# Attention's product with v in plain fp32 on two column halves of the array, with one copy of the turned probabilities

## The chip, the cores and the metric

The kernel runs on one core of one Trainium2 chip. What is measured is the time of the device for one execution, in microseconds (us). TensorE (PE in the profile) multiplies; its weight loads are listed apart as PEld. VectorE is DVE, ScalarE is ACT, GpSimd is POOL, and SyncE (SP) issues nearly all of the transfers.

## The reference

Three stages follow each other. The change is in the first.

```python
# attention: q, k, v are (4, 8, 576, 64); blocks of 64, a block sees itself and what is before it
scores = 1.0 / np.sqrt(D) * np.matmul(q, k.transpose(0, 1, 3, 2))
scores = np.where(block_i >= block_j, scores, -1000000000.0)
attn = np.exp(scores - np.max(scores, axis=-1, keepdims=True))
attn = attn / (np.sum(attn, axis=-1, keepdims=True) + 1e-09)
x = np.matmul(attn, v)                      # then as (2304, 512)
# first feed-forward: w_in (512, 2048), w_out (2048, 512)
h = x @ w_in
x = np.maximum(0.01 * h, h) @ w_out
# second: a skip score, 8 experts, each token to its best expert
y[mask] = gate_w[mask, None] * (np.maximum(xc[mask] @ w1[e], 0.0) @ w2[e])
out[do_compute] = xc + y
```

## The kernel before

**Numbers.** Most products are made of three matmuls in the type F32R: a value is split into a high part (a copy to F32R) and a low part (the value minus the high part), and high by high, high by low and low by high are added in PSUM. The products of the experts' first layer (L1431) and of the gate (L1369) are plain fp32 instead.

**Units and steps.** The 32 heads go in 16 pairs. A pair has 9 units: four query tiles of 128 rows of its first head, one unit with the last 64 rows of both heads (TAIL), four tiles of the second head. The tile number qt (0 to 3) has 128 x (qt + 1) key columns. There are 144 units and 156 steps (STEPS), and at each step s every engine does its part of some unit: PE the scores of unit s + 2 and the transposes of unit s - 2, DVE the row maximum of s, ACT the exponential of s, and ACT and DVE take the transposed probabilities of unit s - 3 out of PSUM. Each engine runs its list in order; all waits are semaphores.

**The path of the probabilities.** `transposes(u)` writes the probabilities, keys on partitions, to one of two banks of `ps_t`. `high_p` (L822 to L828) copies them on ACT to `pt_hi`, and `low_p` (L963 to L966) writes `pt_lo`, bank minus `pt_hi`, on DVE. The bank is free for unit u + 2 after that. Both tiles exist once, so `high_p` waits at some units for the products of the pair before (L825, L826).

**The products with v.** `p_v` (L1265 to L1288) multiplies v (weights, 128 keys by 128 columns) with the turned probabilities (moving, up to 320 query columns). `v_hi` and `v_lo` hold, for each head, its 64 columns beside 64 zero columns, so that the two heads' matmuls with full width add into the same bank `ps_o`, one head into partitions 0 to 63, the other into 64 to 127. Queries are cut in two halves: columns 0 to 255 (two key tiles) and 256 to 575 (five key tiles, the last with 64 rows). The table P_V gives the steps: for pair p at its step 8 and at steps 1, 3, 4, 5, 6 of the next pair. `high_v` on ACT and `low_v` on POOL split v, which is loaded to `v_raw`.

**The row sums.** After a pair, `invert` on DVE adds 1e-9 and takes the reciprocal, PE turns it (L1293), DVE copies it out (`copy_inverse`), SP stores it to memory and spreads it back (`store_inverse`, `spread_inverse`), and POOL multiplies (`normalise`) what `copy_o` took out of `ps_o`. Then ACT and POOL split the result into the input of the first feed-forward.

**Hidden work.** FILL puts groups of the first feed-forward's matmuls (`hidden(g)`, twelve of 384 columns each) behind PE's work of the steps from 50 on: 16 groups at steps 50 to 83, 32 at 86 to 119, 9 at 122 to 142, and the rest of 64 after step 148. From step 38 on SP also loads w_in.

**SP's list** per pair: at step 2 the loads of k and q of the second head of the next pair (6) and of v (2), at 3 a copy of k and the store of the inverse, at 5 the spreading of the inverse (3), at 6 the loads for a first head (4), at 7 a copy of k.

Of the kernel before, what the change touches and what calls it, by code (L numbers as in the profile page):

```python
# [15 lines left out]
P = 128  # L16
# [16 lines left out]
QT = 5  # L33
# [10 lines left out]
P_V = {8: (0, 0, 0, 6), 1: (1, 0, 0, 6), 3: (0, 1, 0, 8), 4: (0, 1, 8, 15), 5: (1, 1, 0, 8), 6: (1, 1, 8, 15)}  # L44
# [31 lines left out]
def fill_steps():  # L76

    at = {s: [] for s in range(STEPS)}
    for g in range(N_ATT_HID):
        if g < FC:  # L80
            at[50 + 34 * g // FC].append(g)
        elif g < 3 * FC:
            at[86 + 34 * (g - FC) // (2 * FC)].append(g)
        elif g < TWO_BANKS:
            at[122 + 5 * (g - 3 * FC) // 2].append(g)
        else:
            at[N_UNITS + 5 + g - TWO_BANKS].append(g)
    return at

# [28 lines left out]
def build(nc, q_t, k_t, v_r, w_in, w_out, w_gs, w1, w2, out):  # L118
    ctx = ExitStack()
    with ctx:  # L120
# [151 lines left out]
        s_v = sem("s_v")  # L272
# [5 lines left out]
        s_vhi = sem("s_vhi")  # L278
        s_vlo = sem("s_vlo")
# [4 lines left out]
        s_pthi = sem("s_pthi")  # L284
        s_ptlo = sem("s_ptlo")
# [59 lines left out]
        N_FULL, N_CONST = 7, 11  # L345
# [43 lines left out]
        def split_done(u):  # L389

            p, i = divmod(u, UNITS)
            return 10 * p + i + 1 + (i > TAIL)

        def pt_views(u):

            i = u % UNITS
            if i == TAIL:
                src = t_bank(u, P, 0, BANK).rearrange("p (k h q) -> p h k q", k=4, h=2)
                return [[src] + [t[:, :, PT_B:PT_W].rearrange("p h (k c) -> p h k c", k=4)[:, :, :, A_COLS:B_COLS]
                                 for t in (pt_hi, pt_lo)]]  # L400
            h, qt = (0, i) if i < TAIL else (1, i - TAIL - 1)
            if qt < 2:
                src = t_bank(u, P, 0, P * (qt + 1))
                views = [[src] + [t[:, h, P * qt:P * qt + P * (qt + 1)] for t in (pt_hi, pt_lo)]]
                if i == TAIL + 1:
                    src = t_bank(u, D, P, 2 * P).rearrange("p (h q) -> p h q", h=2)
                    views.append([src] + [t[0:D, :, TAIL_COL:TAIL_COL + D] for t in (pt_hi, pt_lo)])
                return views
            src = t_bank(u, P, 0, P * (qt + 1)).rearrange("p (k q) -> p k q", q=P)
            return [[src] + [t[:, h, PT_B:PT_W].rearrange("p (k c) -> p k c", k=4)[:, 0:qt + 1, P * (qt - 2):P * (qt - 1)]  # L410
                             for t in (pt_hi, pt_lo)]]


        V_PARTS = ((P, 0, QT - 1), (D, QT - 1, QT))
# [39 lines left out]
        def load_v(e, p):  # L454
            b, hp = p // KC, p % KC
            full = (QT - 1) * P
            if p >= 1:
                e.wait_ge(s_vlo, 2 * p)
            e.dma_start(v_raw[:, 0:QT - 1, :],
                        v_r[b, 0:full, hp * P:(hp + 1) * P].rearrange("(t p) c -> p t c", p=P)).then_inc(s_v, 16)  # L460
            e.dma_start(v_raw[0:D, QT - 1, :], v_r[b, full:S, hp * P:(hp + 1) * P]).then_inc(s_v, 16)
# [3 lines left out]
        def _(e):  # L465
# [75 lines left out]
            for s in range(STEPS):  # L541
                p, i = divmod(s, UNITS)
                if p < N_PAIRS:
                    if i == 2 and p + 1 < N_PAIRS:
                        load_head(e, 2 * p + 3)
                        load_v(e, p + 1)
                    if i == 3 and p + 1 < N_PAIRS:
                        copy_k(2 * p + 2)
                    if i == 6 and p + 2 < N_PAIRS:
# [12 lines left out]
                for g in FILL.get(s - 1, ()):  # L562
                    store_hidden(g)
            for g in FILL[STEPS - 1]:
                store_hidden(g)
            e.wait_ge(s_h, N_ATT_HID)
            e.wait_ge(s_pv, 4 * N_PAIRS)
# [40 lines left out]
        def _(e):  # L608
# [18 lines left out]
            for i in range(2):  # L627
                e.memset(v_hi[i][:, :, 1, :].bitcast(F32), 0.0).then_inc(s_const, 1)
                e.memset(v_lo[i][:, :, 1, :].bitcast(F32), 0.0).then_inc(s_const, 1)
            e.memset(ident[:, :], 0.0).then_inc(s_const, 1)  # L630
            e.wait_ge(s_const, N_FULL)
            for i in range(2):
                e.memset(q2[i][D:P, DM:QW].bitcast(F32), 0.0).then_inc(s_const, 1)
                e.memset(k2[i][D:P, DM:S].bitcast(F32), 0.0).then_inc(s_const, 1)

# [10 lines left out]

            def low_v(p):
                i = p % 2
                for n, (rows_, t0, t1) in enumerate(V_PARTS):
                    e.wait_ge(*before[0])  # L650
                    e.wait_ge(s_vhi, 2 * p + n + 1)
                    before[0] = s_vlo, 2 * p + n + 1
                    e.tensor_tensor(v_lo[i][0:rows_, t0:t1, 0:3:2, :],
                                    v_raw[0:rows_, t0:t1, :].rearrange("p t (g c) -> p t g c", g=2),
                                    v_hi[i][0:rows_, t0:t1, 0:3:2, :].bitcast(F32), ALU.subtract).then_inc(s_vlo, 1)
# [29 lines left out]
            low_v(0)  # L685
            for s in range(STEPS):
# [6 lines left out]
                if i == 2 and 1 <= p < N_PAIRS:  # L693
                    low_v(p)
                if i == 8 and 1 <= p <= N_PAIRS:
# [89 lines left out]
        def _(e):  # L785
# [16 lines left out]
            def high_v(p):  # L802
                i = p % 2
                e.wait_ge(s_v, 32 * (p + 1))
                if p >= 2:
                    e.wait_ge(s_pv, 4 * (p - 1))
                for rows_, t0, t1 in V_PARTS:
                    e.activation(v_hi[i][0:rows_, t0:t1, 0:3:2, :],
# [665 lines left out]
```

## Time and profile before

| | |
|---|---|
| median of three runs | 859.65 us (858.75 to 859.67) |
| profiled execution | 856.37 us, of which the trace spans 854.5 us |
| PE busy | 810.5 us, 95% |
| PEld busy | 736.9 us, 86% |
| DVE, ACT, POOL busy | 414.2, 359.7, 196.8 us |
| granted clock of TensorE, mean | 0.98 |

An engine is counted as busy from an instruction's start to its end, waits in its pipeline among it; matmuls overlap, so the distance from start to start says what one costs, and its duration does not. The attention stage ends at about 360 us.

### The profile page before, as it was taken

How to read it: one execution, taken by the hardware profiler on the slowest of the kernel's cores; microseconds unless marked ns; L12 is line 12 of the kernel's file. 1: busy time of each engine (PE TensorE's matmuls, PEld its weight loads, DVE VectorE, ACT ScalarE, POOL GpSimd, SP SyncE). 2: the span in 40 equal slices, each digit the busy share in tenths (PEclk: the TensorE clock that was granted, in tenths of full speed). 3: DMA queues.
4: the chain of work that ended last, by engine and by line, in shares of the span. 5: the costliest groups of instructions: out<-in, count | busy, mean ns of one | idle time of the engine just before them, and what ended most of it. 6: DMA issues, size and time to landing. Idle time of an engine off the chain costs nothing.

```text
span 854.5 us, 14147 instructions
## 1 busy us (share of the span) xinstructions
PE 810.5 (95%) x4885; PEld 736.9 (86%) x4885; DVE 414.2 (48%) x835; ACT 359.7 (42%) x850; POOL 196.8 (23%) x226
## 2 busy tenths in 40 slices
PE   4889999999999999999999999999999589999999
PEld 3778899999999999899998888888888489888887
DVE  4777766664334456402335455555553232344464
ACT  4677767665445566423442222221221031333353
POOL 5354666433213224110010000000000141221221
PEclk9999799999999999999999999999999879999999
DMA  6444466744453343136666655655561137577740
GB/s 149 132 122 136 142 186 195 203 126 141 118 146 112 105 137 105 50 98 193 173 180 182 190 148 172 182 180 145 168 186 50 38 113 248 174 216 233 227 135 3
DMA packets 101545, 126.82 MB, mean 148 GB/s; under 512 B 15986, under 2 KB 62210, under 8 KB 101480
## 3 DMA queue, kind: packets, MB, share of 16 engines
q1 hardware_dynamic: 98392, 121.33, 48.3%
q0 software_dynamic: 2000, 3.77, 1.4%
q10 hardware_dynamic: 1088, 0.89, 0.5%
q8 instruction: 37, 0.61, 0.3%
q14 instruction: 28, 0.23, 0.1%
HBM read 92.58 MB, written 31.57 MB: 145 GB/s over the span
## 4 chain that ended last, share of the span: by engine, by line
PE 89%; DVE 4%; issue 3%; ACT 3%; DMA 1%; POOL 0%; SPq 0%; DVEq 0%; ACTq 0%; POOLq 0%
PE ps_hid L1431 11%; PE ps_o L1286 9%; PE ps_h L1310 8%; PE ps_x L1345 8%; PE ps_x L1347 8%; PE ps_h L1312 8%; PE ps_h L1311 8%; PE ps_x L1346 8%; PE ps_t L1262 4%; PE ps_y L1442 3%; PE ps_y L1443 3%; PE ps_y L1444 3%; PE ps_s L1247 2%; PE ps_s L1248 2%; PE ps_s L1237 1%
## 5 line engine op out<-in xcount | busy, mean ns | idle before, releaser
L966 DVE TENSOR_TENSOR pt_lo<-ps_t,pt_hi 128x512 fp32r<-128x512 f32 (+4 forms) x160 | 76.5, 486 | 147.1 <-ACT pt_hi L828 146.8
L1310 PE MATMUL ps_h<-xh,win_h 128*128 128x384 f32 x384 | 132.8, 346 | 1.3 <-ACT act L839 1.0
L1311 PE MATMUL ps_h<-xl,win_h 128*128 128x384 f32 x384 | 128.8, 335 | 0.0
L1312 PE MATMUL ps_h<-xh,win_l 128*128 128x384 f32 x384 | 128.7, 335 | 0.0
L1345 PE MATMUL ps_x<-wout_h,g_hi 128*128 128x512 f32 x288 | 116.3, 404 | 0.0
L1347 PE MATMUL ps_x<-wout_h,g_lo 128*128 128x512 f32 x288 | 112.9, 392 | 0.0
L1346 PE MATMUL ps_x<-wout_l,g_hi 128*128 128x512 f32 x288 | 112.1, 389 | 0.0
L1431 PEld LDWEIGHTS ps_hid<-rows_t,w_sb 128*128 128x128 f32 x768 | 89.5, 196 | 8.8 <-issue 8.4
L1431 PE MATMUL ps_hid<-rows_t,w_sb 128*128 128x128 f32 x768 | 91.0, 281 | 5.1 <-PE ps_y L1444 4.2
L839 ACT ACTIVATE act<-ps_h 128x384 f32<-128x384 f32 x96 | 47.1, 491 | 110.1 <-PE ps_h L1312 108.4
L819 ACT ACTIVATE prob<-ps_s,neg_max 128x128 f32<-128x128 f32 (+2 forms) x144 | 78.9, 548 | 25.7 <-DVE neg_max L960 25.2
L828 ACT ACTIVATE pt_hi<-ps_t 128x512 fp32r<-128x512 f32 (+4 forms) x160 | 67.6, 434 | 50.3 <-PE ps_o L1286 31.4
L643 POOL TENSOR_TENSOR k_st<-k_raw,k_st 64x576 fp32r<-64x576 f32 x32 | 45.9, 1433 | 161.6 <-DVE k_st L946 151.1
L1262 PE MATMUL ps_t<-ident,prob 128*128 128x128 f32 x384 | 70.5, 288 | 5.3 <-DVE pt_lo L966 5.3
L1310 PEld LDWEIGHTS ps_h<-xh,win_h 128*128 128x128 f32 x384 | 72.1, 188 | 3.8 <-ACT act L839 1.7
L1003 DVE TENSOR_TENSOR g_lo<-g_raw,g_hi 128x512 fp32r<-128x512 f32 x72 | 49.5, 687 | 52.2 <-ACT g_hi L849 52.2
L960 DVE TENSOR_REDUCE neg_max<-ps_s 128x1 f32<-128x128 f32 (+2 forms) x144 | 72.4, 503 | 0.6 <-PE ps_s L1248 0.5
L1286 PE MATMUL ps_o<-pt_hi,v_hi 128*128 128x320 f32 (+3 forms) x224 | 69.6, 311 | 2.7 <-DVE o_f L988 2.7
L1311 PEld LDWEIGHTS ps_h<-xl,win_h 128*128 128x128 f32 x384 | 72.2, 188 | 0.0
L1312 PEld LDWEIGHTS ps_h<-xh,win_l 128*128 128x128 f32 x384 | 72.1, 188 | 0.0
L1286 PE MATMUL ps_o<-pt_hi,v_lo 128*128 128x320 f32 (+3 forms) x224 | 68.6, 306 | 0.0
L1286 PE MATMUL ps_o<-pt_lo,v_hi 128*128 128x320 f32 (+3 forms) x224 | 66.1, 295 | 0.0
(154 smaller groups left out, 1422.3 us busy)
## 6 DMA issues: line engine op xcount, KB each, us to landing
w_sb<-in_w SPq DMA_DIRECT2D x64, 512.0 KB, 5.2
hidden<-act SPq DMA_DIRECT2D x96, 192.0 KB, 2.2
g_raw<-hidden SPq DMA_DIRECT2D x72, 256.0 KB, 4.5
k_raw<-in_k_t SPq DMA_DIRECT2D x62, 144.0 KB, 2.9
q_raw<-in_q_t SPq DMA_DIRECT2D x32, 144.0 KB, 2.9
x2rows<-x SPq DMA_DIRECT2D x18, 256.0 KB, 2.4
out<-x SPq DMA_DIRECT2D x18, 256.0 KB, 2.6
k<-k_st SPq DMA_DIRECT2D x31, 144.0 KB, 2.7
```

The source lines that it names most:

```text
L819: e.activation(prob_of(u), score_out(u), ACT.Exp, bias=neg_max[:, u % 4:u % 4 + 1], scale=1.0, accum_out=row_sum[p % 2][:, i:i + 1]).then_ ...
L960: e.tensor_reduce(out=neg_max[:, u % 4:u % 4 + 1], in_=src, axis=AX.XY if u % UNITS == TAIL else AX.X, op=ALU.max, negate=True).then_inc(s ...
L966: e.tensor_tensor(lo, src, hi.bitcast(F32), ALU.subtract).then_inc(s_ptlo, 1)
L1262: last = e.transpose(t_bank(u, P, P * kt, P * kt + P), tile[:, P * kt:P * kt + P], ident[:, :])
L1286: last = e.matmul(ps_o[:, a:a + cols], stat, (pt_hi, pt_lo, pt_hi)[j][0:kr, h, at:at + cols], start=h == 0 and n == 0, stop=h == 1 and n = ...
L1310: e.matmul(dst, win_h[:, f, kc, :], xh[slot][:, kc, :], start=kc == 0, stop=False)
L1311: e.matmul(dst, win_h[:, f, kc, :], xl[slot][:, kc, :], start=False, stop=False)
L1312: last = e.matmul(dst, win_l[:, f, kc, :], xh[slot][:, kc, :], start=False, stop=kc == KC - 1)
L1345: e.matmul(dst, hi, wout_h[:, f, :], start=f == 0, stop=False)
L1346: e.matmul(dst, hi, wout_l[:, f, :], start=False, stop=False)
L1347: last = e.matmul(dst, lo, wout_h[:, f, :], start=False, stop=f == FC - 1)
L1431: last = e.matmul(ps_hid[half][:, P * f - HALF * half:P * (f + 1) - HALF * half], w1_sb[i][:, c, P * f:P * f + P], rows_t[:, c, :], start= ...
```

## The change

The two heads of a pair no longer share full-width matmuls with zero columns. Each product with v is one matmul in plain fp32 with 64 weight columns, the first head into partitions 0 to 63 of `ps_o`, the second into 64 to 127, one after the other for each key tile. v is used as it was loaded (`v_sb`, two buffers), and the splits `high_v` and `low_v` go. The turned probabilities are copied once, to `pt` (two buffers, one a pair), by ACT for units 3 and 8 of a pair and by DVE for the others. The last key tile uses all 128 rows; the unused ones are set to zero once.

With it: the products are at steps 1, 3 and 4 of the next pair (P_V has three entries, both heads in each); the transposes have a third bank, `ps_h1`, up to unit 44, before the first hidden group needs it; hidden groups are cut in two parts that FILL places apart; the second `copy_o` is at step 5 instead of 7, `normalise` at 7 instead of 8; SP issues the loads of v at step 5, ahead of the spreading; the addition of 1e-9 is on ACT (step 8); ACT's copy of a hidden group stands ahead of the exponential of the step.

```diff
-P_V = {8: (0, 0, 0, 6), 1: (1, 0, 0, 6), 3: (0, 1, 0, 8), 4: (0, 1, 8, 15), 5: (1, 1, 0, 8), 6: (1, 1, 8, 15)}
+P_V = {1: (0, 0, 2), 3: (1, 0, 2), 4: (1, 2, 5)}
+PT_ACT = (3, 8)
+T3_UNITS = 5 * UNITS
...
-        v_raw = sb("v_raw", [P, QT, P], F32, r2)
-        v_hi = [sb(f"v_hi{i}", [P, QT, 3, D], F32R, r2) for i in range(2)]
-        v_lo = [sb(f"v_lo{i}", [P, QT, 3, D], F32R, r2) for i in range(2)]
+        v_sb = [sb(f"v_sb{i}", [P, QT, P], F32, r2) for i in range(2)]
...
-        pt_hi = sb("pt_hi", [P, 2, PT_W], F32R, r2)
-        pt_lo = sb("pt_lo", [P, 2, PT_W], F32R, r2)
+        pt = [sb(f"pt{i}", [P, 2, PT_W], F32, r2) for i in range(2)]
...
         def t_bank(u, rows_, a, z):
-            c = BANK * (u % 2)
-            return ps_t[0:rows_, c + a:c + z]
+            n = t_index(u)
+            return ps_h1[0:rows_, a:z] if n == 2 else ps_t[0:rows_, BANK * n + a:BANK * n + z]
...
+        def turned_ready(e, u):
+            p = u // UNITS
+            e.wait_ge(s_ptr, u + 1)
+            if p >= 2:
+                e.wait_ge(s_pv, 2 * (p - 1))
...
         def load_v(e, p):
-            if p >= 1:
-                e.wait_ge(s_vlo, 2 * p)
+            if p >= 2:
+                e.wait_ge(s_pv, 2 * (p - 1))
...
                     if i == 2 and p + 1 < N_PAIRS:
                         load_head(e, 2 * p + 3)
-                        load_v(e, p + 1)
...
+                    if i == 5 and p + 1 < N_PAIRS:
+                        load_v(e, p + 1)
...
+            def add_epsilon(p):
+                rs = row_sum[p % 2]
+                e.wait_ge(s_exp, UNITS * (p + 1))
+                e.activation(rs[:, :], rs[:, :], ACT.Copy, bias=1e-9).then_inc(s_eps, 1)
...
-            def low_p(u):
-                e.wait_ge(s_pthi, split_done(u))
-                for src, hi, lo in pt_views(u):
-                    e.tensor_tensor(lo, src, hi.bitcast(F32), ALU.subtract).then_inc(s_ptlo, 1)
+            def copy_turned(u):
+                turned_ready(e, u)
+                for src, dst in pt_views(u):
+                    e.tensor_copy(dst, src).then_inc(s_ptd, 1)
...
+            def p_v(p, half, first, end):
                 if first == 0:
+                    turned(e, UNITS * p + (TAIL + 2, UNITS - 1)[half])
+                    e.wait_ge(s_v[p % 2], 32 * (p // 2 + 1))
+                    if p + half >= 1:
+                        e.wait_ge(s_of, 2 * p + half)
+                    if half:
+                        e.wait_ge(s_invt, p + 1)
...
-                    stat = (v_hi, v_hi, v_lo)[j][i][0:kr, kt, h:h + 2, :].rearrange("p g c -> p (g c)")
-                    last = e.matmul(ps_o[:, a:a + cols], stat, (pt_hi, pt_lo, pt_hi)[j][0:kr, h, at:at + cols],
-                                    start=h == 0 and n == 0, stop=h == 1 and n == len(steps) - 1)
+                    for h in range(2):
+                        own = slice(D * h, D * h + D)
+                        last = e.matmul(ps_o[own, a:a + cols], v_sb[p % 2][:, kt, own], pt[p % 2][:, h, at:at + cols],
+                                        start=kt == 0, stop=kt == tiles - 1)
```

## Rows read from the trace of the kernel before

**Rows 1.** Windows cut at L1293: us, then PE, PEld, DVE, ACT, POOL busy, clock, DMA.

```profile
28.90:45.60 16.70, 13.64 (x93) 11.77 (x93) 12.46 (x29) 11.60 (x34) 5.71 (x5) 1.00 0.45 126
45.60:62.30 16.70, 14.91 (x93) 13.27 (x93) 12.45 (x29) 11.60 (x34) 7.63 (x8) 0.90 0.45 125
...
79.00:96.80 17.80, 15.61 (x93) 13.35 (x92) 13.03 (x29) 12.59 (x36) 10.48 (x10) 0.86 0.60 171
96.80:118.70 21.90, 21.01 (x128) 19.91 (x129) 13.34 (x31) 15.53 (x44) 12.44 (x11) 0.88 0.58 165
...
238.60:268.30 29.70, 29.52 (x190) 28.53 (x190) 12.83 (x28) 15.43 (x43) 7.72 (x7) 1.00 0.43 124
```

**Rows 2.** Chain of waits, 45 to 63 us: start, us, engine, what.

```profile
46.54 0.77 PE ps_s L1237 x4
...
55.40 0.61 ACT pt_hi L828
...
61.06 0.90 DVE row_sum L971
```

**Rows 3.** Waits of the whole span: total us, times, longest us.

```profile
ACT pt_hi L828 <- PE ps_o L1286: 31.4, 29, 2.0
```

**Rows 4.** PE in order of time (start, us): from three bursts of products with v.

```profile
143.22 0.39 PE L1286 MATMUL ps_o<-pt_hi,v_hi 128*128 128x320 f32 x1
...
144.47 0.28 PE L1247 MATMUL ps_s<-k_st,q_hi 128*128 128x256 f32 x1
...
254.40 0.39 PE L1286 MATMUL ps_o<-pt_hi,v_lo 128*128 128x320 f32 x1
...
254.83 0.27 PE L1286 MATMUL ps_o<-pt_hi,v_lo 128*128 128x192 f32 x1
255.03 0.29 PE L1286 MATMUL ps_o<-pt_hi,v_hi 64*128 64x64 f32 x1
...
255.48 0.44 PE L1310 MATMUL ps_h<-xh,win_h 128*128 128x384 f32 x1
...
261.00 0.36 PE L1286 MATMUL ps_o<-pt_hi,v_hi 128*128 128x256 f32 x1
...
261.73 0.39 PE L1310 MATMUL ps_h<-xh,win_h 128*128 128x384 f32 x1
```

**Rows 5.** Plain fp32: L1431 on the page, and two stretches of PE's order.

```profile
L1431 PE MATMUL ps_hid<-rows_t,w_sb 128*128 128x128 f32 x768 | 91.0, 281 | 5.1 <-PE ps_y L1444 4.2
...
742.90 7.41 PE L1431 MATMUL ps_hid<-rows_t,w_sb 128*128 128x128 f32 x64 [0.58 <-PE ps_y L1444]
...
502.76 0.96 PE L1369 MATMUL ps_gate<-wg,x2t 128*128 128x9 f32 x8
```

**Rows 6.** Weight loads (PEld) of the same burst as 255.03 in rows 4.

```profile
255.03 0.18 PEld L1286 LDWEIGHTS ps_o<-pt_hi,v_hi 64*128 64x128 f32 x1
255.14 0.19 PEld L1286 LDWEIGHTS ps_o<-pt_lo,v_hi 64*128 64x128 f32 x1
```

**Rows 7.** PE around a transpose with 64 weight columns, and that one's load.

```profile
257.70 0.22 PE L1247 MATMUL ps_s<-k_st,q_hi 128*128 128x128 f32 x1
...
257.87 0.28 PE L1260 MATMUL ps_t<-ident,prob 128*64 128x128 f32 x1
...
257.83 0.11 PEld L1260 LDWEIGHTS ps_t<-ident,prob 128*64 128x64 f32 x1
```

**Rows 8.** Groups of ACT and DVE in 28.9 to 79 us: busy us, mean ns.

```profile
L828 ACT ACTIVATE pt_hi<-ps_t 128x512 fp32r<-128x512 f32 (+4 forms) x30 | 12.6, 430 | 6.4 <-PE ps_o L1286 4.5 <-PE ps_t L1262 1.6
...
L971 DVE TENSOR_SCALAR row_sum<-row_sum 128x9 f32<-128x9 f32 x3 | 2.9, 966 | 0.0
```

**Rows 9.** SP's issues in order of time around the store of an inverse.

```profile
49.32 0.58 SPq L468 DMA_DIRECT2D k<-k_st  x1
49.94 0.50 SPq L472 DMA_DIRECT2D inverse<-inv_t  x1
51.95 0.45 SPq L480 DMA_DIRECT2D inv_all<-inverse  x1
```

More of the change, by code:

```diff
@@ L79, in fill_steps, with filled_at, t_index, t_before @@
     for g in range(N_ATT_HID):
[L80 to L87, printed above, removed]
-    return at
+        for part in range(2):
+            n = 2 * g + part
+            if g < FC:
+                s = 50 + 34 * n // (2 * FC)
+            elif g < 3 * FC:
+                s = 86 + 34 * (g - FC) // (2 * FC)
+            elif g < TWO_BANKS:
+                s = 122 + 22 * (n - 6 * FC) // (2 * (TWO_BANKS - 3 * FC))
+            else:
+                s = N_UNITS + 5 + g - TWO_BANKS
+            at[s].append((g, part))
+    return at
+def filled_at(s):
+    return [g for g, part in FILL.get(s, ()) if part]
+def t_index(u):
+    return u % 3 if u < T3_UNITS else u % 2
+def t_before(u):
+    return next((v for v in range(u - 1, max(u - 4, -1), -1) if t_index(v) == t_index(u)), None)
 FILL = fill_steps()
@@ L271, in build @@
         s_qk = [sem(f"s_qk{i}") for i in range(2)]
-        s_v = sem("s_v")
+        s_v = [sem(f"s_v{i}") for i in range(2)]
         s_khi = sem("s_khi")
@@ L645, in low_k @@
                 before[0] = s_klo, n + 1
[L647 to L655, printed above, removed]
             def normalise(p):
@@ L684, in _ @@
             low_k(1)
-            low_v(0)
             for s in range(STEPS):
@@ L692, in _ @@
                         low_k(2 * p + 3)
-                if i == 2 and 1 <= p < N_PAIRS:
-                    low_v(p)
-                if i == 8 and 1 <= p <= N_PAIRS:
+                if i == 7 and 1 <= p <= N_PAIRS:
                     normalise(p - 1)
@@ L1014, in _ @@
                     maximum(s)
-                if 3 <= s < N_UNITS + 3:
-                    low_p(s - 3)
+                if 3 <= s < N_UNITS + 3 and (s - 3) % UNITS not in PT_ACT:
+                    copy_turned(s - 3)
                 if p + 1 < N_PAIRS:
@@ L1293, in turn_inverse, with hidden, hidden_waits @@
                 e.transpose(ps_o[0:UNITS, B_COLS:B_COLS + P], inv[:, :], ident[:, :]).then_inc(s_invp, 1)
-            def hidden(g):
+            def hidden(g, part):
                 m, f = divmod(g, FC)
                 slot = m % 4
+                dst = ps_hidden(g)
+                if part == 0:
+                    hidden_waits(g)
+                for kc in range(KC // 2 * part, KC // 2 * (part + 1)):
+                    e.matmul(dst, win_h[:, f, kc, :], xh[slot][:, kc, :], start=kc == 0, stop=False)
+                    e.matmul(dst, win_h[:, f, kc, :], xl[slot][:, kc, :], start=False, stop=False)
+                    last = e.matmul(dst, win_l[:, f, kc, :], xh[slot][:, kc, :], start=False, stop=kc == KC - 1)
+                if part:
+                    last.then_inc(s_h, 1)
+            def hidden_waits(g):
+                m, f = divmod(g, FC)
+                if g == 0:
+                    turned(e, T3_UNITS - 1)
                 if f == 0:
@@ L1307, in hidden @@
                     e.wait_ge(s_act, g)
-                dst = ps_hidden(g)
-                for kc in range(KC):
-                    e.matmul(dst, win_h[:, f, kc, :], xh[slot][:, kc, :], start=kc == 0, stop=False)
-                    e.matmul(dst, win_h[:, f, kc, :], xl[slot][:, kc, :], start=False, stop=False)
-                    last = e.matmul(dst, win_l[:, f, kc, :], xh[slot][:, kc, :], start=False, stop=kc == KC - 1)
-                last.then_inc(s_h, 1)
             scores(0)
@@ L1322, in _ @@
                 p, i = divmod(s, UNITS)
-                if i in P_V:
-                    pair = p if i == 8 else p - 1
-                    if 0 <= pair < N_PAIRS:
-                        p_v(pair, *P_V[i])
-                    if i == 1 and 1 <= p <= N_PAIRS:
-                        turn_inverse(pair)
-                for g in FILL[s]:
-                    hidden(g)
+                if i in P_V and 1 <= p <= N_PAIRS:
+                    p_v(p - 1, *P_V[i])
+                    if i == 1:
+                        turn_inverse(p - 1)
+                for g, part in FILL[s]:
+                    hidden(g, part)
             for g in range(N_ATT_HID, N_HID):
-                hidden(g)
+                for part in range(2):
+                    hidden(g, part)
             def project(k):
```

119 lines of the change are left out of this document (48 added, 71 removed).

## The prediction

> **What bounds the kernel now.** I read the windows table first, cut at the instruction of L1293 that turns a pair's inverse row sums (one per pair of heads). Pairs without hidden work inside them take 16.70 us, whether the granted clock is 1.00 or 0.90 [rows 1]; so TensorE's speed does not set them, although PE counts as busy for 13.6 to 14.9 us. A pair that also holds the first projection's matmuls (238.6 to 268.3 us) has PE busy for all but 0.2 us [rows 1]: there the order of PE's instructions is the time. The attention stage has two halves with different limits; the border is step 50 of 144.
>
> The chain of waits of one early pair shows the loop of the first half: the scores of the tail unit (46.54), then PE alone through the steps with four bursts of products with v until ACT's pt_hi copy at 55.40, then ACT and DVE to the end of row_sum at 61.96 and one maximum and exponential more [rows 2]. That is 8.8 us on PE and 7.9 on ACT and DVE, in series: 16.7. The wait in the middle exists because pt_hi is a single buffer; all waits of that kind come to 31.4 us [rows 3].
>
> **What the products with v cost now.** At full clock a burst of eight F32R products of 320 columns starts at 143.22 and the next instruction at 144.47: 1.25 us. The second kind (one product of 320, three of 192, three of 64) takes 254.40 to 255.48, 1.08 us; the short one 261.00 to 261.73, 0.73 us [rows 4]. A pair has each twice: 2 x 3.06 = 6.12 us. The hidden matmuls beside them are untouched (the same 64 groups, cut in halves).
>
> **The new products.** Over its seven key tiles a head has 384 + 960 + 192 + 64 = 1600 columns. Plain fp32 stands in the expert stage: a loop body has 32 such products (4 chunks by 8 blocks), the row says x64, so two records a product; 7.41 us less the last one's tail of 0.17 is 113 ns a record of 128 columns [rows 5]. Are that the weights or the columns? The gate's eight records of only 9 columns follow at (0.96 - 0.25) / 7 = 0.10 us [rows 5], so weights alone explain most of it, and 0.88 ns a column is only an upper bound; the lower is F32R's 1.25 us / (8 x 320) = 0.49 [rows 4]. I take 0.875: a 128-column F32R record whose weights are in lasts 0.22 us [rows 7], an fp32 one 0.281 [rows 5], longer by just another 128 columns at F32R's rate, so the columns pass twice. One head: 1600 x 2 x 0.875 = 2.8 us (1.6 at the lower bound).
>
> The heads now fill partitions 0 to 63 and 64 to 127 of ps_o from the two column halves of the array. No row shows two halves at work together, so I bound it. Side by side without loss: 2.8 us, and 0.7 us for the first record of each of three bursts, which has no partner: 3.5. In series: 5.6. Weights are loaded one ahead (255.14, under the matmul of 255.03 [rows 4, 6]), so a partner starts late by one small load, about 0.08 us (a 64-column load lasts 0.11 [rows 7]); 14 such offsets are 1.1 us. Then the change of shape. Where a burst goes from 128 rows to 64, the next matmul starts 0.20 us after the last instead of 0.11, and its load only then, at 255.03 [rows 4, 6]: a gap of 0.09 us, and another one back. The change removes all four of a pair, since the last key tile now uses 128 rows. The column change, in contrast, is free where it can be seen: the load for 64 columns starts at 257.83, under running matmuls, and its transpose 0.04 later [rows 7]. So six changes between full and half columns cost between 0 and 6 x 0.09 = 0.5 us. Bounds side by side: 3.5 to 5.1; I take the middle, 4.3, since neither row is nearer: a saving of 1.8 us a pair (1.0 to 2.6).
>
> The Trainium skill (TensorEngine Tiling (Array Packing), Key Properties) says that changing the tiling mode drains the engine. The trace agrees for 64 rows (0.09 us) and disagrees for the 64-column transposes; the sum would be 0.25 us a pair worse or better by the one or the other.
>
> **Second half, steps 55 to 144.** 9.9 pairs bound by PE: 9.9 x 1.8 = 17.8 us. Waits of ACT for the single pt_hi buffer (31.4 us in all, 1.5 in each early pair [rows 3, 8]) are mostly hidden here; I give 2 us for them. Sum 20. DVE and ACT stay cover: busy 12.8 and 15.4 of 29.7 us [rows 1]. Halving a hidden group adds no instruction; its copy moves ahead of the exponential on ACT, which PE needs only two steps later.
>
> **First half, steps 0 to 55.** What leaves ACT: ten pt_hi copies, 4.2 us a pair [rows 8], of which two of 0.6 stay, and v_hi. What leaves DVE: ten subtractions become eight copies (0.69 each for the two of 512 that leave; I price a copy like the subtraction, since both read the same bank), and row_sum's addition, 0.97 a pair [rows 8], goes to ACT. POOL loses low_v. New floors of a pair:
> - DVE: 12.45 [rows 1] - 1.4 - 1.0 = 10.1.
> - PE's issue: scores 3.7, 25 transposes x 0.11 = 2.8, products 4.3: 10.8 (12.6 before).
> - SP: an issue comes 0.62 us after another [rows 9]; 18 of them (10 for q and k, 2 for v, 2 copies of k, 1 + 3 of the inverse) are 11.2. It also stands from 50.44 to 51.95 until the inverse has landed [rows 9]; load_v moves into exactly that place and covers 1.2 of the 1.5. Floor 11.5. load_v's new wait, for the products of the pair before last, is over by then; behind it are the spreading and the loads of q and k.
> - The loop of [rows 2], redone: from the tail scores PE goes through two bursts instead of four (1.3 + 0.4 + 0.4 + 1.4 + 0.6 + 0.9, 5.0), then comes o_f's second copy, moved from step 7 to 5, and DVE's steps 5 to 10, some 5.8 us by the durations of its maxima, copies and q, then the exponential, 0.9: 11.7. The pt_hi waits go, through two buffers and the third transpose bank (up to unit 44). A new wait of PE, the second burst for inv_t (DVE, step 2), ends just before the o_f copy that it waits for anyway: 0; behind it stand the scores and transposes of the step after, due two steps later.
>
> Three limits of 11.7, 11.5 and 10.8 do not overlap perfectly; I take 12.6. Start to step 10, 18.1 us: -3.7. Three pairs: 3 x 4.1 = 12.3. 79.0 to 96.8, where SP also loads w_in (22.5 issues, 14.0): 17.8 to 14.6, -3.2. 96.8 to 118.7, with three hidden groups of 2.1 on PE (10.8 + 6.3, with friction 17.8): -4.1 [rows 1]. Sum 23.3; with 15.0 a pair 12, with 11.7 a pair 28.
>
> The start is not touched: transfers of q and k set it, not the memsets that are exchanged. The stages after attention hold the same instructions.
>
> **The sum.** 20 + 23.3 = 43.3. The profiled execution took 856.4 us, hence 813.1; the median of the runs is 3.3 us above it, hence 816.4.
>
> **Rivals.**
> - *The halves do not run together* (0.22). Products 5.6 + 0.5 = 6.1 a pair: the second half gains only its 2 us. In the first half PE issues 12.6 a pair and the loop is 11.7 + 1.6, with friction 14.3: 2 + 3 x 2.4 + 1.5 + 1.3 = 12. Time 859.65 - 14 = 846. For it: no row shows two products at once. Against: the next weights are taken under a running matmul everywhere, and the halves share neither weights nor columns nor partitions of ps_o; that puts it below the forecast. The Trainium skill (TensorE: Matmul & The Clock Gate, Part 3, Measured speedup vs the span model) gives 2.38x for three column tiles; no run here shows it.
> - *The products gain, the first half does not* (0.07): landings of SP's transfers hold early pairs at 15.5. Gain 20 + 6: 834.
> - *Slower* (0.08): a half-column load is not accepted under a running matmul. Each of the 56 records pays its load, at least 0.11 us [rows 7]: 5.6 + 6.2 = 11.8 a pair, 5.7 x 9.9 = 56 in the second half, and with PE at 18.3 a pair 8 in the first: about 924. It decides from where a pair's products exceed 7.3 us (6.1 + 12 / 9.9). Against it: among 64-row products the load starts under the matmul before [rows 6]. The Trainium skill (TensorE: Matmul & The Clock Gate, Part 3, The mechanism) states that a load overlaps a matmul in flight only if its row group differs; here the row group is the same in both halves, and by that rule this rival would be the forecast. The full-width rows of this trace disagree with it.
> - *A lower clock* (inside the range): it is 0.90 and 0.86 in early pairs with PE at 75% of its issue time [rows 1]. A denser PE should not be granted less; at 0.75 there, 6 to 8 us come back.
>
> **How the numbers follow.** 0.63 for the forecast, own range 803 to 832 (products 3.5 to 5.1: +-8; first half +5 to -11). 0.22 at 846, 0.07 at 834, 0.08 slower. The range reaches to the first rival: 803 to 848. A difference of 0.2% (1.7 us) is about what a measurement of this kernel tells from none. Faster 0.89, same 0.03, slower 0.08.
>
> **What would show it.** In the changed trace the products with v have 64 columns and two records each; if the heads overlap, a burst of two key tiles of 320 for both heads lasts 1.2 to 1.5 us, in series 2.3. Early pairs last 12 to 13.5 us with SP nearly without gaps; the pair of 238.6 to 268.3 lasts 27.9 instead of 29.7; no engine waits for ps_o ahead of a turned copy. Bursts over 2.5 us, or a granted clock under 0.9 in the second half, would make it wrong.

## The result, and the profile after

| | before | after |
|---|---|---|
| median | 859.65 us (858.75 to 859.67) | 824.39 us (823.04 to 827.12) |
| profiled execution, its span | 856.37, 854.5 us | 823.04, 821.3 us |
| PE, PEld busy | 810.5, 736.9 us | 773.3, 672.1 us |
| DVE, ACT, POOL busy | 414.2, 359.7, 196.8 us | 382.9, 307.6, 165.8 us |
| granted clock, mean | 0.98 | 0.98 |

The ratio is 0.9596 [0.9571, 0.9621]: 35.3 us less, where 43.3 were forecast. The time is inside the range of 803 to 848 us and inside the forecast's own range, 8.0 us above the predicted 816.4. The span of the profiled executions shrank by 33.2 us. Cut where the prediction cut it, the parts are (us):

| part | forecast | measured |
|---|---|---|
| steps 0 to 55 | -23.3 | 118.7 to 105.0: -13.7 |
| step 55 to the end of the first feed-forward's hidden work | -20 | 327.1 to 308.2: -18.9 |
| what follows | 0 | -0.6 |

So the second half came within 1.1 us of the forecast, and 9.6 us of the first half did not come. By parts, the first half saved 2.2 us up to the first cut (forecast 3.7), then 5.3, 1.6, 0.6, 2.7 and 1.3 in its five pairs (forecast 4.1, 4.1, 4.1, 3.2 and 4.1). In what follows, the early pairs are the first four of these; the fifth is the first pair with hidden work.

From the page of after, the chain by engine and the group of the turned copies on DVE:

```profile
PE 87%; DMA 4%; SPq 4%; issue 2%; DVE 2%; ACT 1%; POOL 0%; POOLq 0%; DVEq 0%; ACTq 0%
...
L968 DVE COPY pt<-ps_t 128x256 f32<-128x256 f32 (+4 forms) x113 | 49.3, 444 | 107.5 <-PE ps_t L1261 107.5
```

SP's queue (SPq) and DMA have 4% each of the chain. The copies of the turned probabilities wait for PE's transposes (107.5 us idle before them) and not for the products. The same stands in the list of waits, whose ACT row answers to [rows 3]: the 31.4 us of ACT's waits for ps_o ahead of a turned copy are gone.

```profile
ACT pt L863 <- PE ps_t L1261: 27.4, 13, 3.6
...
PE ps_s L1236 <- DMA k<-k_st: 9.6, 4, 2.8
```

The second row is new: four times, near the start of the second, third, fourth and fifth pair, PE's scores wait for the transfer of the copy of k, 9.6 us in all. The windows, cut as in [rows 1] at the instruction that turns a pair's inverse row sums (now L1294; columns us, then busy PE, PEld, DVE, ACT, POOL, clock, DMA share, GB/s):

```profile
38.00:53.10 15.10, 12.31 (x80) 8.85 (x78) 10.24 (x26) 8.44 (x25) 5.36 (x6) 0.89 0.49 136
53.10:69.20 16.10, 12.43 (x81) 8.72 (x79) 10.32 (x26) 8.44 (x25) 6.34 (x6) 0.89 0.47 133
69.20:84.30 15.10, 12.47 (x80) 9.08 (x78) 10.21 (x24) 9.25 (x27) 6.79 (x7) 0.89 0.62 174
...
218.70:246.60 27.90, 27.60 (x178) 24.70 (x176) 10.63 (x25) 11.94 (x33) 5.83 (x5) 1.00 0.46 132
```

The pair with hidden work takes 27.9 us, the forecast's number. Of the early pairs the first takes 11.4 us (26.6 to 38.0) and the next 15.1, 16.1 and 15.1, where 12.6 (14.6 for the fourth) were forecast. DVE has 10.2 to 10.3 us in them (forecast 10.1) and ACT 8.4 to 9.3: neither is the limit. The chain of waits of two of them, where [rows 2] had ACT and DVE behind PE:

```profile
37.15 3.00 DMA k<-k_st
40.15 0.09 issue
40.24 0.76 PE ps_s L1236 x4
...
42.84 2.03 PE ps_o L1287 x8
...
45.63 1.15 PE ps_o L1287 x12
46.79 0.02 issue
46.80 0.38 SPq L483
...
52.27 3.89 DMA k<-k_st
56.16 0.09 issue
56.25 0.76 PE ps_s L1236 x4
...
58.07 2.30 PE ps_o L1287 x8
```

It can be read as a loop. (A burst is the products with v of one step.) From the tail unit's scores (L1236) PE goes on to the last burst of the pair (45.63 to 46.78); SP's load of v (L483) starts 0.02 us behind that burst's end; behind it come the other issues of SP, the last of them the copy of k at 52.27. Its data lands 3.89 us later, and only then can the next tail unit's scores start. SP stood still for it, as its issues show (start, us):

```profile
43.32 0.51 SPq L496 DMA_DIRECT2D inverse<-inv_t  x1
46.80 0.38 SPq L483 DMA_DIRECT2D v_sb<-in_v_r  x1
...
52.27 0.59 SPq L492 DMA_DIRECT2D k<-k_st  x1
```

From 43.83 to 46.80 nothing is issued. All such waits of SP are one row of its list:

```profile
SPq L483 <- PE ps_o L1287: 21.3, 11, 3.5
```

### The profile page after: what moved, and what is told of

Same layout as the page of the kernel before. It is cut to its first block, busy times and chain, and to the rows that moved or that the text cites. A ratio compares the mean times of both kernels' runs of the same rounds, so it can differ in the third digit from the quotient of the medians.

```text
span 821.3 us, 13529 instructions
## 1 busy us (share of the span) xinstructions
PE 773.3 (94%) x4661; PEld 672.1 (82%) x4661; DVE 382.9 (47%) x787; ACT 307.6 (37%) x706; POOL 165.8 (20%) x196
## 4 chain that ended last, share of the span: by engine, by line
PE 87%; DMA 4%; SPq 4%; issue 2%; DVE 2%; ACT 1%; POOL 0%; POOLq 0%; DVEq 0%; ACTq 0%
PE ps_hid L1439 11%; PE ps_h L1303 9%; PE ps_x L1353 8%; PE ps_x L1355 8%; PE ps_x L1354 8%; PE ps_h L1305 8%; PE ps_h L1304 8%; PE ps_o L1287 6%; PE ps_t L1261 3%; PE ps_y L1450 3%; PE ps_y L1451 3%; PE ps_y L1452 3%; PE ps_s L1246 2%; DMA k<-k_st 2%; PE ps_s L1247 2%
## 5 line engine op out<-in xcount | busy, mean ns | idle before, releaser
L1303 PE MATMUL ps_h<-xh,win_h 128*128 128x384 f32 x384 | 136.5, 355 | 3.4 <-ACT act L838 2.8
L968 DVE COPY pt<-ps_t 128x256 f32<-128x256 f32 (+4 forms) x113 | 49.3, 444 | 107.5 <-PE ps_t L1261 107.5
L826 ACT ACTIVATE prob<-ps_s,neg_max 128x128 f32<-128x128 f32 (+2 forms) x144 | 78.3, 546 | 10.4 <-DVE neg_max L962 10.2
L1355 PEld LDWEIGHTS ps_x<-wout_h,g_lo 128*128 128x128 f32 x288 | 54.1, 188 | 12.0
L1354 PEld LDWEIGHTS ps_x<-wout_l,g_hi 128*128 128x128 f32 x288 | 54.3, 189 | 10.1
L1261 PE MATMUL ps_t<-ident,prob 128*128 128x128 f32 x344 | 61.5, 282 | 0.7 <-ACT prob L826 0.7
L1353 PEld LDWEIGHTS ps_x<-wout_h,g_hi 128*128 128x128 f32 x288 | 54.2, 188 | 9.7
L848 ACT ACTIVATE g_hi<-g_raw 128x512 fp32r<-128x512 f32 x72 | 43.6, 626 | 49.2 <-DVE g_raw L997 40.9
```

The lines of the kernel that those rows point to most:

```text
L826: e.activation(prob_of(u), score_out(u), ACT.Exp, bias=neg_max[:, u % 4:u % 4 + 1], scale=1.0, accum_out=row_sum[p % 2][:, i:i + 1]).then_ ...
L968: e.tensor_copy(dst, src).then_inc(s_ptd, 1)
L1261: last = e.transpose(t_bank(u, P, P * kt, P * kt + P), tile[:, P * kt:P * kt + P], ident[:, :])
L1303: e.matmul(dst, win_h[:, f, kc, :], xh[slot][:, kc, :], start=kc == 0, stop=False)
L1353: e.matmul(dst, hi, wout_h[:, f, :], start=f == 0, stop=False)
L1354: e.matmul(dst, hi, wout_l[:, f, :], start=False, stop=False)
```

## How long the products take now

PE in order of time in the pair of 218.7 to 246.6 (start, us):

```profile
224.36 0.41 PE L1261 MATMUL ps_t<-ident,prob 128*128 128x128 f32 x2
224.70 1.30 PE L1287 MATMUL ps_o<-pt,v_sb 128*64 128x320 f32 x8
225.93 0.39 PE L1246 MATMUL ps_s<-k_st,q_hi 128*128 128x256 f32 x1
...
226.28 0.49 PE L1261 MATMUL ps_t<-ident,prob 128*128 128x128 f32 x3
226.70 1.20 PE L1287 MATMUL ps_o<-pt,v_sb 128*64 128x320 f32 x12
227.83 0.44 PE L1303 MATMUL ps_h<-xh,win_h 128*128 128x384 f32 x1
```

From start to start the burst of two key tiles takes 225.93 - 224.70 = 1.23 us, inside the 1.2 to 1.5 named for overlapping heads, and the last burst 227.83 - 226.70 = 1.13; the third, of the pair's first kind, takes 0.80. That is 3.16 us a pair, against 6.12 before and 4.3 forecast. The eight records of the first start at 0.000, 0.007, 0.320, 0.327, 0.589, 0.596, 0.858 and 0.865 us: always two together, one of each head, and the next two 0.269 us later. With 320 columns that is 0.84 ns a column and record (forecast 0.875), and a full-width record of 320 columns takes the same 0.269 us by itself (239.07 to 240.96 in the full-width kernel below, seven such distances).

## Experiments

### The load of v two steps later

Theory W: load_v's wait for PE closes the loop above, because the copy of k stands behind it. Rival L: the landings of SP's transfers, or SP's own issues, hold the pair, wherever load_v stands.

```diff
-                    if i == 5 and p + 1 < N_PAIRS:
-                        load_v(e, p + 1)
...
                         copy_k(2 * p + 3)
+                        load_v(e, p + 1)
```

> The changed kernel with load_v issued after the second copy of k (step 7) instead of at step 5. Theory W (SP's wait for the products of the pair before, ahead of the spreading, four loads and a copy of k, closes the loop of the early pairs): that wait is over at step 7, the early pairs go from 15.1 to 16.1 us to about 12.5, 5 pairs give 12 to 14 us: about 811 us. Theory L (landings of 3 us and the bandwidth of the transfers hold the early pairs, whatever the order): within 3 us of the changed kernel, 821 to 825.

Measured: 818.43 us (814.2 to 821.95), ratio 0.9538 [0.9492, 0.9584]. Early pairs 11.4, 13.2, 12.8 and 15.2 us in place of 11.4, 15.1, 16.1 and 15.1. The loop is gone from the second and third. In the fourth the chain goes again from a burst of products (61.39) to the load of v (62.21), now at its new place. W stands in two pairs, while the median lies between W's 811 and L's 821. The single times go with the mean granted clock: 814.2 and 815.5 us at 0.985, 822.0 and 821.4 at 0.977 and 0.979.

### Three buffers of v, the load at the changed kernel's place

The move above changes the place of two issues as well as the wait. Here the place stays and the wait goes, as the buffer it asks for has been free for a pair.

```diff
-        v_sb = [sb(f"v_sb{i}", [P, QT, P], F32, r2) for i in range(2)]
+        v_sb = [sb(f"v_sb{i}", [P, QT, P], F32, r2) for i in range(3)]
...
-            if p >= 2:
-                e.wait_ge(s_pv, 2 * (p - 1))
+            if p >= 3:
+                e.wait_ge(s_pv, 2 * (p - 2))
```

> The changed kernel with three buffers of v, so that load_v at its place at step 5 waits for the products of one pair earlier. Theory W: the wait goes, the issues stay where they are; the same as with the late load, about 811 us, or up to 2 us better since the load still covers the landing of the inverse. Theory P (not the wait but the 1.2 us of issues and the transfer of v at that place matter): no gain here, 821 to 825, although the late load gains. Theory L: 821 to 825 for both.

Measured: 816.74 us (815.37 to 820.1), ratio 0.9514 [0.9477, 0.9551], early pairs 12.3, 13.2, 12.9 and 13.0. It is the wait and not the place, though the 811 us of the expectation were missed by 5.7: the fifth pair takes 22.6 us, 1.9 more than in the changed kernel. Two early pairs in the windows view, and the chain of one of them:

```profile
37.70:50.80 13.10, 10.71 (x80) 7.92 (x78) 10.12 (x26) 8.45 (x25) 6.20 (x6) 1.00 0.62 174
50.80:63.70 12.90, 10.81 (x81) 7.98 (x79) 10.22 (x26) 8.33 (x25) 6.29 (x6) 1.00 0.58 163
```

```profile
39.52 0.76 PE ps_s L1237 x4
...
41.34 1.23 PE ps_o L1288 x8
...
47.59 1.41 POOL k_st L669
49.01 0.07 issue
49.07 1.90 POOL inv_all L677
...
51.43 0.35 ACT xh L813
51.77 0.46 ACT prob L827 x2
52.23 0.14 issue
52.37 0.76 PE ps_s L1237 x4
```

Two things are to be seen. The clock is 1.00 where it was 0.89, and the same eight records that took 2.03 and 2.30 us in the chain of after take 1.23 here. From the tail scores to the end of the last burst PE needs 44.46 - 39.52 = 4.94 us, and in the changed kernel, behind an idle stretch of 2.8 us, 62.83 - 56.25 = 6.58. The lower clock thus made that loop longer by 1.6 us of the 16.05 (45.63 to 61.68) that it took; 14.4 are left, against 12.85 here (39.52 to 52.37). The kernel with two banks below, which keeps the wait, splits the rest further. And the next limit shows: POOL's normalisation (L677), then ACT's split of its result (L813), which stands ahead of the exponential that the tail scores wait for.

### The split of x out of that place

High_x (ACT) and low_x (POOL), the two halves of x's split, go from steps 0 and 1 to step 2, on top of three buffers of v.

```diff
-                if i == 1 and 2 <= p <= N_PAIRS + 1:
+                if i == (1 if p > N_PAIRS else 2) and 2 <= p <= N_PAIRS + 1:
                     low_x(p - 2)
...
-                if i == 0 and 2 <= p <= N_PAIRS + 1:
+                if i == (0 if p > N_PAIRS else 2) and 2 <= p <= N_PAIRS + 1:
                     high_x(p - 2)
```

> The kernel with three buffers of v, and ACT's and POOL's splitting of the attention output (high_x, low_x) moved from steps 0 and 1 to step 2 of the second pair after, except for the last pair. In the chain of the three-buffer kernel the early pairs (12.9 us) go through POOL's low_k (1.41) and normalise (1.90), then high_x on ACT, which stands ahead of the exponentials that the tail scores wait for. Theory: that wait is what is late next; out of the way, the early pairs go to 11.5 to 12.2 us, 3 to 5 us off the whole, 812 to 814. Rival: SP's 18 issues (11.2 us) and the landing of the inverse hold them at 12.9: 816 to 818.

Measured: 813.97 us (813.66 to 814.6), ratio 0.9484 [0.946, 0.9509], faster than the changed kernel and the one with three buffers. The total came as expected, but not where it was expected: the early pairs take 11.3, 13.7, 12.0 and 14.8, together no less than with three buffers alone (51.8 against 51.3), and the gain is in the first pair with hidden work, 17.7 (after 20.7, three buffers 22.6). Part of that may be the clock, which is at its lower level from 79.2 to 86.0 us with three buffers and never in this pair here. Steps 0 to 55 now end at 95.8 instead of 118.7: 22.9 us, where the prediction had 23.3. Its sum for the first half was attainable, on another order of the queues than the changed kernel has.

### Both heads' weights at full width

Theory H: the column halves run side by side, and that carries the second half's gain. Rival F: the gain is that of plain fp32 (two records for three products, and no gap for 64 rows). Here all 128 columns of v are the weights for either head; the two heads' contributions are added over all 128 partitions of ps_o, so the output of attention is not the reference's. Number and width of the moving records are those of the changed kernel.

```diff
-                        last = e.matmul(ps_o[own, a:a + cols], v_sb[p % 2][:, kt, own], pt[p % 2][:, h, at:at + cols],
-                                        start=kt == 0, stop=kt == tiles - 1)
+                        last = e.matmul(ps_o[:, a:a + cols], v_sb[p % 2][:, kt, :], pt[p % 2][:, h, at:at + cols],
+                                        start=kt == 0 and h == 0, stop=kt == tiles - 1 and h == 1)
```

> The changed kernel, but each product with v keeps all 128 columns of v as weights and writes all 128 partitions of ps_o, the two heads added into each other: the attention output is not the reference's, the number and size of the moving columns is that of plain fp32 without column halves. If the halves work side by side (pairs of records start 7 ns apart in the trace), the burst of four products of 320 goes from 1.23 to 2.2 us, a pair's products from 3.15 to 5.6, less 0.4 for the entries that need no change of shape: +2.0 us a pair, 20 us in the second half and up to 10 in the first, about 854 us. If the start times only show queueing and the halves run in series anyway: within 3 us of 824.

Measured: 851.18 us (849.71 to 852.78), ratio 0.9912 [0.9881, 0.9943]. The pair that took 27.9 us takes 29.8 (29.7 before), and its bursts last 1.31, 1.91 and 2.09 us from start to the next start:

```profile
239.07 2.32 PE L1287 MATMUL ps_o<-pt,v_sb 128*128 128x320 f32 x8
240.99 0.52 PE L1246 MATMUL ps_s<-k_st,q_hi 128*128 128x256 f32 x1
...
241.80 2.28 PE L1287 MATMUL ps_o<-pt,v_sb 128*128 128x320 f32 x12
243.89 0.42 PE L1303 MATMUL ps_h<-xh,win_h 128*128 128x384 f32 x1
```

The 5.31 us of bursts are 95% of the 5.6 that the prediction had for the heads in series (and a little short: the scores start 0.03 us behind the last record of the burst of 1.91, and the next start comes 0.36 us later, where it is 0.22 in the changed kernel). All of the gain in the second half hangs on the halves (step 55 to the end of the hidden work: 328.5 us, against 327.1 before and 308.2 after); what is left of the gain lies mainly in the first, which ends at 111.2 instead of 118.7. H stands, and F is out for the second half.

### All key tiles of the first head first

Same products, but within a burst head 0's key tiles come before head 1's, so a partner is further back in PE's queue. If records start strictly in order, nothing can overlap but at the border of the heads; if each half takes its own records as they come, nothing changes.

```diff
-                for kt in range(first, end):
+                for h, kt in [(h, kt) for h in range(2) for kt in range(first, end)]:
...
-                    for h in range(2):
```

> The changed kernel with all key tiles of the first head ahead of all of the second in each burst, the same products otherwise. If the array takes records strictly in order and only neighbours on different halves overlap: the burst of 1.23 us becomes about 2.0 (only one place where the heads meet), and the whole about 20 to 28 us slower, 844 to 852. If each half has a queue of its own that is served ahead of order, 1.23 us stays and the time is within 2 us of 824.

Measured: 831.19 us (828.88 to 832.11), ratio 0.9664 [0.9633, 0.9695], between the two expectations; both were wrong. The bursts of two key tiles are unchanged (0.81 and 1.23 us), that of three is 1.71 instead of 1.13:

```profile
231.89 1.79 PE L1286 MATMUL ps_o<-pt,v_sb 128*64 128x320 f32 x12
233.60 0.45 PE L1302 MATMUL ps_h<-xh,win_h 128*128 128x384 f32 x1
```

In the shorter bursts the first record of head 1 starts 0.013 us behind the first of head 0, though three older records of head 0 stand ahead of it. In the burst of twelve five stand ahead at first. Its records differ in their columns (320, 320, 192, 192, 64, 64 for each head), so the heads can be told apart: head 1's first did not start with head 0's second record (0.320 us in, four older ones left) but with its third (0.589; head 1's at 0.595), when three were left. So records of the other half start out of order, past three older ones in all three bursts and past four in none.

### The last key tile on 64 rows

The prediction priced the change of rows at 0.09 us each way and took its removal into the sum. Here it is put back.

```diff
+                    kr = D if kt == QT - 1 else P
...
-                        last = e.matmul(ps_o[own, a:a + cols], v_sb[p % 2][:, kt, own], pt[p % 2][:, h, at:at + cols],
+                        last = e.matmul(ps_o[own, a:a + cols], v_sb[p % 2][0:kr, kt, own], pt[p % 2][0:kr, h, at:at + cols],
```

> The changed kernel with the last key tile on 64 rows, as before the change. By the gap of 0.09 us in the trace of before, the third burst gets one change of rows inside and is 0.09 us longer (1.22 instead of 1.13) and the whole 1 to 2 us slower. If a change of shape costs what the entry to the half columns costs (0.17 us), 1.30 us. If it is free once the columns are halved already, 1.13.

Measured, in one execution: the burst of three key tiles takes 1.28 us instead of 1.13.

```profile
233.07 1.34 PE L1288 MATMUL ps_o<-pt,v_sb 128*64 128x320 f32 x12
234.35 0.44 PE L1304 MATMUL ps_h<-xh,win_h 128*128 128x384 f32 x1
```

That is 0.15 us a pair, 1.5 us over the ten pairs that PE bounds. It has two parts: the first record on 64 rows starts 0.26 us behind the one before it instead of 0.16, which is 0.10 for the change of rows, close to the 0.09 of the prediction; and the second record on 64 rows follows in 0.107 us instead of 0.055. The whole execution took 832.31 us, but no total can be read from it: the granted clock was 0.76 from 40 to 80 us, where the changed kernel has 0.87 and 0.88.

### Two banks for the transposes

The third bank is a part of the change that the prediction needed in the redone loop, together with the second pt.

```diff
-T3_UNITS = 5 * UNITS
+T3_UNITS = 0
```

> The changed kernel without the third bank for the transposes (two banks throughout). The prediction took the third bank for part of what loosens the early loop. If it carries some of the first half's gain, the early pairs become 0.5 to 1.5 us longer each, 827 to 830; if the wait in SP's list sets these pairs, the bank is worth nothing, 822 to 826.

Measured: 821.27 us (817.18 to 825.84), ratio 0.9585 [0.9547, 0.9624]. The interval covers that of the changed kernel, and the early pairs are not longer (11.3, 13.6, 13.7, 13.8). The third bank brings nothing that can be measured. Its early pairs are shorter than 15.1 and 16.1 although load_v still waits, and the chain says why. Its second loop, and the row of its waits:

```profile
43.51 1.15 PE ps_o L1287 x12
...
50.14 3.13 DMA k<-k_st
...
53.38 0.76 PE ps_s L1236 x4
...
57.19 1.15 PE ps_o L1287 x12
```

```profile
PE ps_s L1236 <- DMA k<-k_st: 9.5, 4, 3.3
```

This is the loop of the changed kernel at full clock (1.00 from 40 to 80 us, where the changed kernel has 0.87 and 0.88). It takes 13.68 us (43.51 to 57.19) against 16.05 there and 12.85 without the wait. From the tail scores to the last burst PE takes 3.81 us instead of 5.43, and the copy of k lands in 3.13 instead of 3.89: these two are the difference of 2.4. So the wait itself costs 0.8 us a loop. And PE stands waiting for k as long as in the changed kernel (9.5 and 9.6 us), while the clock fell in three places from 40 to 80 us there and in none here.

### The hidden copy behind the exponential

The prediction gave this move neither a cost nor a gain. Its argument was about the exponential, which the copy now delays and which PE needs only two steps later.

```diff
-                for g in filled_at(s - 1):
-                    copy_hidden(g)
                 if s < N_UNITS:
...
                     high_w_in(f)
+                for g in filled_at(s - 1):
+                    copy_hidden(g)
```

> The changed kernel with ACT's copy of a hidden group behind the exponential of the step again. The prediction gave the new place nothing. Then 822 to 826. If the earlier copy is what frees the only bank of the hidden groups in time, PE waits for it in each of the 32 groups of the steps 86 to 119, about 0.3 us each: 830 to 834.

Measured: 831.06 us (825.56 to 833.57), ratio 0.9691 [0.9654, 0.9729], 6.7 us over the changed kernel by the medians and 2.5 by the fastest execution of each. The wait that the move had removed is back:

```profile
PE ps_h L1303 <- ACT act L838: 8.9, 14, 2.6
```

In the changed kernel the same row reads 2.8 us, 10 times, longest 0.9. The difference is not in steps 86 to 119 but where hidden work begins and ends: the first pair with it takes 26.3 us instead of 20.7. In that pair PE waits 3.6 us for ACT's copy, and 2.8 more for POOL's low half of w_in, a wait that the changed kernel does not have; whether the later copy brings that about isn't settled. Part of the 6.7 is clock (0.971 to 0.983 here, 0.975 to 0.981 there), and how much isn't separated. The earlier copy brought something, by a number that these runs leave open.

## Why the prediction was right, and where it was not

**The products: the sum right, by luck.** The forecast saved 1.8 us a pair, and the pair of 218.7 to 246.6 fell by 29.7 - 27.9 = 1.8. But the bursts take 3.16 us, below even the lower bound of 3.5 and 1.1 below the value taken. Mis-sized were the partner's offset (0.08 us taken, 0.007 measured) and the lone first record, which isn't lone: its partner starts with it, although each has its own weights to load. On the other side stand waits that were not in the sum. From a group of transposes to the next start the trace has these rows, in the changed kernel:

```profile
239.12 0.38 PE L1261 MATMUL ps_t<-ident,prob 128*128 128x128 f32 x2
...
239.62 0.19 PEld L1303 LDWEIGHTS ps_h<-xh,win_h 128*128 128x128 f32 x1 [0.36 <-ACT act L838]
```

The hidden group waits 0.36 us for ACT's copy of the hidden group before it. In the kernel before, a burst with v stood at this place and covered that wait: it started 0.03 us behind the last transpose. With the distances of all nine groups of transposes in a pair added up, PE has 0.82 us in them before and 1.74 now: 0.37 more from this one place, 0.04 from another, and 0.17 more at each of the three entries into a burst (0.20 us instead of 0.03). Of this 0.17, 0.08 is there with plain fp32 at full width (0.11 in the full-width kernel), and 0.09 is the change to half columns, the upper end of the prediction's "between 0 and 6 x 0.09". Saved in bursts 2.96, lost around transposes 0.92, lost elsewhere 0.2 (0.11 of it in the scores behind a burst): 1.8. The middle of the bounds was met because two errors of about one size stood against each other. (The lower bound was itself a little low: three lone first records of 320, 320 and 256 columns at 0.875 ns are 0.78 us, not 0.7.)

**The rows.** The row change was priced at 0.09 us from full-width rows; inside the halves it measured 0.10, and 0.05 more for the second record on 64 rows.

**Side by side or in series.** The forecast's 0.63 against 0.22 was decided as it said. The trace confirms what spoke against the serial rival, and the full-width kernel shows the serial case: 851.18 us, where the rival was given 846.

**A load under a running matmul.** The rival "slower" does not occur. Couples of 320 columns follow one another in 0.269 us with both their next loads (0.13 to 0.14 us each) under them. The prediction priced this rival too high: a pair has 28 records (7 key tiles, 2 heads, 2 records each; the bursts above have 8, 8 and 12), not 56, so by its own terms a pair's products would have taken 5.6 + 3.1 = 8.7 us and not 11.8, and the second half would have lost 26 us and not 56. That is still slower. By the sentence of the Trainium skill (TensorE: Matmul & The Clock Gate, Part 3, The mechanism) that the prediction names, these loads would have waited, since both halves use the same row group; this case's trace does not agree with it. The same section also lets a load into the background weight buffer go ahead of running matmuls, with which the trace can be squared.

**The step that failed** is in the first half: "load_v's new wait, for the products of the pair before last, is over by then". At SP's step 5 of pair p the load is for pair p + 1 and takes the buffer of pair p - 1, whose products run at steps 1, 3 and 4 of pair p. So it is the burst just ahead that it waits for, not one a pair back. The prediction named what is queued behind it, the spreading and the loads of q and k, and left out the copy of k, whose transfer the tail scores need. That closes another loop, PE to SP to DMA to PE, which the list of limits (11.7, 11.5, 10.8) did not have. With three buffers of v, which take this wait out, steps 0 to 55 end at 99.2 instead of 105.0, and the median is 7.65 us lower, where the forecast was 8.0 too low. Not all of this is the wait itself. At full clock it costs 0.8 us a loop (13.68 against 12.85), and single executions at the same mean clock differ by 2 to 4 us: 817.18 (two banks, wait kept) against 815.37 (three buffers) at 0.987, 820.17 against 817.12 at 0.983, 824.45 (changed kernel) against 820.1 at 0.979. The rest of the 7.65 went with the clock. The fifth pair's miss (20.7 where 17.8 was forecast) is not the wait's: three buffers did not shorten it, and it took 17.7 only when the split of x had moved.

**The limits themselves.** DVE's 10.1 was measured at 10.2. The loop of 11.7, with 12.6 taken for friction (14.6 in the fourth pair), held on average once the wait and the split of x were out of it: 11.3, 13.7, 12.0 and 14.8. The rival "the first half does not gain" had 15.5 us a pair and a chance of 0.07; the pairs took 15.1 to 16.1, through transfers behind SP indeed, though its time of 834 was missed, since the first pairs and the pairs with hidden work gained all the same. It deserved more weight: a landing of 2.7 us for a copy of k, behind a queue of 0.62 us issues, stood on the page of before. (The range of the forecast does not follow from its terms at the upper end: 8 for the products and 11 for the first half lead from 816.4 to 835, not 832.)

**The lower clock.** "A denser PE should not be granted less" held with three buffers of v from 37.7 to 63.7 us (1.00) and not in the changed kernel (0.89 in three early pairs). Its premise was not met there: PE was not denser, it stood idle for 1.9 to 2.8 us a time, waiting for the copy of k. But that idle time alone does not decide: the kernel with two banks stands idle for 2.0 to 2.1 us at the same places of three pairs and kept 1.00 up to 83 us. What decides between the two isn't shown. Where the clock was lower, it cost 1.6 us of a loop on PE, twice the price of the wait.

**Priced at nothing.** The third bank: right, nothing. The hidden copy ahead of the exponential: given nothing, it brought a gain. The argument looked at what the move delays and not at what it brings earlier, the copy that the next hidden group waits for. The forecast had no gain for it, so in the sum it worked against the failed step.

## What to carry to other kernels

When a load is moved in a queue, write down for that very step which iteration's work it waits for and everything behind it up to the next thing that the bound engine needs; a wait that is one iteration nearer than assumed turns a spare queue into a loop. Products that fill only half of the columns pay best in couples, one of each half, next to each other in the order of issue. And look at what a burst of work covers: if the next group on that engine is waiting for another engine meanwhile, as the hidden groups do for ACT's copy, moving the burst away gives back part of its saving.

## What the runs showed of the hardware

- Two plain fp32 matmuls on the two column halves start 0.007 us apart and run together at the rate of one: a couple of 320-column records in 0.269 us, two such full-width ones in 0.54 (0.269 each).
- A record of the other half can start ahead of three older ones, and did not while four stood ahead of it (heads_outer).
- A change from 128 to 64 rows inside the halves costs 0.10 us, about the 0.09 at full width.
- From the last transpose to a burst of products 0.03 us pass for F32R at full width, 0.11 for plain fp32 at full width and 0.20 for plain fp32 on the halves.
- Behind PE's idle stretch of 2.8 us in an early pair (53.4 to 56.2 us in the changed kernel), the clock went from its upper level, 2.4 GHz, to its lower one, 1.2 GHz (granted 0.52 and 0.63 in two slices of 2 us that hold some of both), and it came back while PE was busy:

```profile
54.00:56.00 2.00, 0.00 (x0) 0.00 (x0) 1.02 (x2) 1.96 (x6) 1.30 (x3) 1.00 0.61 169
56.00:58.00 2.00, 1.75 (x13) 1.61 (x13) 0.31 (x2) 1.35 (x5) 0.24 (x1) 1.00 0.55 154
58.00:60.00 2.00, 2.00 (x9) 0.75 (x8) 1.54 (x4) 1.32 (x4) 1.40 (x1) 0.52 0.29 64
60.00:62.00 2.00, 2.00 (x11) 1.30 (x11) 0.28 (x1) 0.23 (x2) 0.00 (x0) 0.63 0.12 24
```

- Executions of one kernel spread with the mean granted clock: 814.2 us at 0.985 and 821.95 at 0.977 for the later load of v, against 813.66 to 814.6 at 0.985 to 0.987 for the kernel with three buffers and the split of x moved.
